# A chunked delta-rule attention in front of two MLPs: the head in another order, and the state's products only where the state is in use

## The reference

```
k_n = k / (norm(k) + 1e-06)
state = zeros(B, H, D, D)
for t in range(S):
    y[t]  = q[t] @ state
    v_old = state applied to k_n[t]
    state = state + beta[t] * outer(k_n[t], v[t] - v_old)
# then: mixture of 8 experts (logits = x_norm @ emb_norm.T / tau, one expert a token),
# then: (relu(x @ w_in) ** 2) @ w_out
```

## Time and profile before

| | us |
|---|---|
| median of 3 runs (1204.06 to 1205.07) | 1204.73 |
| the profiled execution, whole | 1206.8 |
| its span, first to last instruction | 1205.0 |
| attention, until about | 432 |
| experts, until about | 780 |
| last MLP, until the end | 1205 |

### The profile page before, as it was taken

The page is one execution under the profiler, slowest core; times in us unless marked ns, Lnnn a source line. Parts: engine busy times, 40 slices in busy tenths (PEclk is TensorE's granted clock), DMA queues, the critical chain, the costliest instruction groups (busy, mean ns, idle before and its releaser), DMA issues. The chain is left out here.

```text
span 1205.0 us, 24540 instructions
## 1 busy us (share of the span) xinstructions
PE 1131.3 (94%) x10176; PEld 971.6 (81%) x10176; DVE 531.2 (44%) x1216; ACT 441.4 (37%) x1038; POOL 369.8 (31%) x319
## 2 busy tenths in 40 slices
PE   2799999999999889999999999689999999999998
PEld 1588888888888777888778877579999999999997
DVE  4688888788887513211111111043433434343332
ACT  2477777676776511110011100033332323233332
POOL 3566667677777511133451000140010100000000
PEclk9999999999999979999999999989999999999999
DMA  6122223333330369999989640120000000000000
GB/s 109 21 41 39 37 37 68 81 81 81 74 81 16 108 251 349 377 368 375 377 284 335 224 156 27 46 79 1 27 27 27 27 1 27 1 27 1 27 1 27
DMA packets 130558, 130.69 MB, mean 108 GB/s; under 512 B 78280, under 2 KB 116880, under 8 KB 130448
## 3 DMA queue, kind: packets, MB, share of 16 engines
q1 hardware_dynamic: 120448, 105.72, 28.9%
q0 software_dynamic: 5536, 17.31, 4.1%
q10 hardware_dynamic: 4464, 6.10, 1.4%
HBM read 129.70 MB, written 21.43 MB: 125 GB/s over the span
## 5 line engine op out<-in xcount | busy, mean ns | idle before, releaser
L1501 PE MATMUL mlp_ps<-xg_t,win 128*128 128x512 f32 x864 | 216.3, 397 | 1.4 <-DVE xg_t L1574 1.4
L1512 PE MATMUL mlp_ps<-wout,sq_hl 128*128 128x384 f32 x1152 | 215.4, 336 | 0.0
L1512 PEld LDWEIGHTS mlp_ps<-wout,sq_hl 128*128 128x128 f32 x1152 | 204.2, 188 | 7.2
L1501 PEld LDWEIGHTS mlp_ps<-xg_t,win 128*128 128x128 f32 x864 | 161.5, 190 | 32.2 <-DVE xg_t L1574 1.8
L1232 PEld LDWEIGHTS expert_ps<-xs_t,w_sb 128*128 128x128 f32 x1488 | 173.5, 194 | 8.9 <-ACT xs_t L1258 1.0
L1232 PE MATMUL expert_ps<-xs_t,w_sb 128*128 128x128 f32 x1488 | 173.8, 277 | 0.6 <-ACT xs_t L1258 0.6
L1242 PE MATMUL expert_ps<-w_sb,ht_sb 128*128 128x384 f32 x496 | 165.1, 486 | 0.0
L1242 PEld LDWEIGHTS expert_ps<-w_sb,ht_sb 128*128 128x128 f32 x496 | 91.8, 190 | 57.5
L1581 DVE TENSOR_TENSOR sq<-relu 128x512 f32<-128x512 f32 x96 | 66.5, 692 | 160.9 <-ACT relu L1539 154.8
L767 DVE TENSOR_TENSOR p_cur<-newt,cst 128x256 f16<-128x256 f32 x288 | 109.0, 420 | 46.8 <-PE newt L413 43.4
L1539 ACT ACTIVATE relu<-mlp_ps 128x512 f32<-128x512 f32 x96 | 57.3, 597 | 171.9 <-PE mlp_ps L1501 171.5
(11 more groups left out here) (199 smaller groups left out, 1577.2 us busy)
## 6 DMA issues: line engine op xcount, KB each, us to landing
w_sb<-in_moe_w SPq DMA_DIRECT2D x62, 1536.0 KB
xs<-sorted_x SPq DMA_DIRECT2D x31, 192.0 KB
sorted_y<-ys ACTq DMA_DIRECT2D x31, 192.0 KB, 5.9
k_raw<-in_k SPq DMA_DIRECT2D x24, 192.0 KB, 3.0
q_pad<-in_q SPq DMA_DIRECT2D x24, 192.0 KB, 3.9
v_raw<-in_v SPq DMA_DIRECT2D x24, 192.0 KB, 4.1
out<-o_sb SPq DMA_DIRECT2D x6, 768.0 KB, 3.5
sorted_x<-zeros SPq DMA_DIRECT2D x11, 384.0 KB, 5.5
```

The lines of the kernel that those rows point to most:

```text
L1501: mm = pe.matmul(ps[:, 4 + f % 2, :], win[:, a, kd, f * P:(f + 1) * P], xg_t[:, par, b, kd], start=(kd == 0 and a + b == 0), stop=(kd == K ...
L1512: mm = pe.matmul(ps[:, t, 0:DM], sq_hl[:, f % RING, a, t * P:(t + 1) * P], wout[:, b, f], start=(f == 0 and a + b == 0), stop=(f == K2 - 1 ...
```

## The change

- SP issues k of tile 0 first, then the constants and beta; after GpSimd's first fill (q_pad, now its first) come q0, k1, v0, the embedding and tau, q1, v1, and the rest. k, q and v have semaphores of their own. Loads of tiles 4 to 7 wait for `s_d1` (v read by `difference`) instead of `s_r0`.
- The embedding's normalization moves into the loops: `norm_emb` and `root_emb` into turn -1, `scale_emb`, `turn_emb` and `keep_emb` into turn 0 (`scale_emb` in front of `first_t(0)`, `keep_emb` in front of `high_rhs(0)`; the two casts of `count_w` go with it).
- `turn(n, 0)` waits for `k_pad` and q, not for `kb_nat`; `update` waits for `kb_nat`.
- `p_cur` is filled in `norm_k(0)`, and only its odd blocks (half the elements). The state is cleared behind `kb_nat(0)` instead of in front of `kb_nat(1)`.
- For tiles 0 to 3 `start_values`, `old_outputs` and `first_rhs` are left out, and v takes the place of rhs. For tiles 20 to 23 `kb_nat`, `update` and `new_state` are left out. Both leave the result as it is, since the state is zero in the one case and unread in the other.

```diff
@@ sync
+        load_k(0)
         sp.dma_start(cst[:, :], consts).then_inc(s_const, 16)
         sp.dma_start(beta_rows[:, :, :], ...).then_inc(s_beta, 16)
+        sp.wait_ge(s_zero, 1)
+        load_q(0)
+        load_k(1)
+        load_v(0)
         sp.dma_start(emb_rows[:, :], emb).then_inc(s_small, 16)
         sp.dma_start(tau_sb[:, 0:1], ...).then_inc(s_small, 16)
+        load_q(1)
+        load_v(1)
...
+            if n < 2 * B:
+                wait(sp, s_d1, n - 3)
+            else:
+                sp.wait_ge(s_r0, n - 3 - B)
@@ gpsimd
-        pool.memset(rt.zeros[:, :], 0.0)
-        for pad in (q_pad, k_pad):
-            pool.memset(pad[:, :, :, :], 0.0)
+        pool.memset(q_pad[:, :, :, :], 0.0).then_inc(s_zero, 1)
+        pool.memset(k_pad[:, :, :, :], 0.0)
         pool.memset(kb_nat[:, :, :, :], 0.0).then_inc(s_zero, 1)
+        pool.memset(rt.zeros[:, :], 0.0).then_inc(s_zero, 1)
...
-            if n == 0:
-                pool.wait_ge(s_setup, 3)
...
+            if n >= NP - B:
+                return
             wait(pool, s_su_ps, n - 3)
             pool.wait_ge(s_kpad, n + 1)
-            if n == 1:
-                pool.memset(state[:, :, :, :], 0.0).then_inc(s_init, 1)
             pool.tensor_tensor(kb_nat[:, n % B, :, 0:D], ...).then_inc(s_kb, 1)
+            if n == 0:
+                pool.memset(state[:, :, :, :], 0.0).then_inc(s_init, 1)
@@ tensor
             if p == 0:
-                pe.wait_ge(s_kb, n + 1)
+                pe.wait_ge(s_kpad, n + 1)
+                pe.wait_ge(s_q_in[n % B], 16 * (n // B + 1))
@@ tensor: start_values and old_outputs; vector: first_rhs
+            if n < B:
+                return
@@ tensor: update; vector: new_state
-            if not there(n):
+            if not there(n) or n >= NP - B:
@@ scalar: square_k
-            act.wait_ge(s_in[n % B], 48 * (n // B + 1))
+            act.wait_ge(s_k_in[n % B], 16 * (n // B + 1))
@@ scalar: high_rhs
+            if n < B:
+                act.wait_ge(s_v_in[n % B], 16)
+                wait(act, s_x1_ps, n)
+                act.copy(rhs_hi[:, :, :], v_raw[:, n % B]).then_inc(s_rhi, 1)
+                return
@@ scalar: the loop
+            if n == -1:
+                root_emb()
...
             newton_tt(n, 6)
+            if n == 0:
+                keep_emb()
             root(n + 3)
+            if n == -3:
+                keep_beta()
             high_rhs(n)
@@ vector: norm_k
-            if n == 1:
+            if n == 0:
+                dve.wait_ge(s_const, 16)
                 for level in range(1, LEVELS):
-                    ins = dve.tensor_copy(p_cur[:, level - 1], ident.unsqueeze(1).to_broadcast([P, H, P]))
+                    own = odd_blocks(ident.unsqueeze(1), level)
+                    ins = dve.tensor_copy(odd_blocks(p_cur[:, level - 1], level),
+                                          own.to_broadcast([P, H] + list(own.shape[2:])))
@@ vector: the loop
             first_rhs(n - 1)
+            if n == -1:
+                norm_emb()
+            if n == 0:
+                scale_emb()
             first_t(n)
```

More of the change, by code:

```diff
@@ L152, in attention @@
     s_small = sem("s_small")
-    s_in = [sem("s_in0"), sem("s_in1"), sem("s_in2"), sem("s_in3")]
-    s_setup = sem("s_setup")
+    s_k_in = [sem(f"s_k_in{b}") for b in range(4)]
+    s_q_in = [sem(f"s_q_in{b}") for b in range(4)]
+    s_v_in = [sem(f"s_v_in{b}") for b in range(4)]
+    s_beta = sem("s_beta")
+    s_beta_ps = sem("s_beta_ps")
+    s_emb_t = sem("s_emb_t")
+    s_count_w = sem("s_count_w")
     s_zero = sem("s_zero")
@@ L321, in difference @@
             pool.wait_ge(s_x1, n + 1)
-            pool.tensor_tensor(d1[:, :, :], rhs[:, :, :], x1[:, :, :], ALU.subtract).then_inc(s_d1, 1)
+            right = v_raw[:, n % B] if n < B else rhs[:, :, :]
+            pool.tensor_tensor(d1[:, :, :], right, x1[:, :, :], ALU.subtract).then_inc(s_d1, 1)
         def low_part(n):
@@ L437, in start_values @@
                 return
+            if n < B:
+                return
             pe.wait_ge(s_t3, 4 * n + 4)
-            wait(pe, s_state, 2 * n)
+            pe.wait_ge(s_state, 2 * min(n, NP - B))
             for p in range(HP):
@@ L493, in new_outputs @@
             pe.wait_ge(s_u, n + 1)
+            if n < B and hf == 0:
+                wait(pe, s_lg, n)
+                pe.wait_ge(s_emb_t, 1)
             for h in range(4 * hf, 4 * hf + 4):
                 mm = pe.matmul(y_ps[:, h * D:(h + 1) * D], aq[:, n % B, h, P:2 * P], u_all[:, h],
-                               start=False, stop=(h == H - 1), skip_group_check=True)
+                               start=(n < B and h == 0), stop=(h == H - 1), skip_group_check=True)
             if hf == 1:
@@ L550, in _ @@
             route(n - 2)
+            if n == 0:
+                turn_emb()
             newton_p(n, 3)
@@ L707, in reciprocal_norm, with norm_emb, scale_emb @@
             dve.wait_ge(sem_in, base + 5)
[L709 to L717 removed]
+        def norm_emb():
+            dve.wait_ge(s_small, 32)
+            dve.tensor_tensor_reduce(out=y_sq[0:E, :], in0=emb_rows[:, :], in1=emb_rows[:, :], scale=1.0, scalar=0.0,
+                                     op0=ALU.mult, op1=ALU.add, accum_out=emb_n[:, 0:1]).then_inc(s_en, 1)
+            dve.reciprocal(tau_sb[:, 1:2], tau_sb[:, 0:1]).then_inc(s_tau, 1)
+            dve.tensor_copy(rt.base[:, :], cst[:, cs.REGION:cs.REGION + E]).then_inc(rt.s_base, 1)
+        def scale_emb():
+            dve.wait_ge(s_en, 2)
+            reciprocal_norm(emb_n[:, 0:1], emb_n[:, 1:2], [emb_n[:, i:i + 1] for i in (2, 3, 4, 5)], s_en, 2)
+            dve.reciprocal(emb_n[:, 6:7], emb_n[:, 5:6]).then_inc(s_tau, 1)
+            dve.wait_ge(s_tau, 2)
+            dve.tensor_scalar(emb_rows[:, :], emb_rows[:, :], emb_n[:, 6:7], tau_sb[:, 1:2], ALU.mult, ALU.mult)\
+               .then_inc(s_en, 1)
         def sum_k(n):
```

95 lines of the change are left out of this document (51 added, 44 removed).

## The result

The changed kernel took 1194.37 us (median of 4 runs, 1193.41 to 1196.90), the kernel before 1204.90 on the same chip (4 runs): 10.5 us faster, a ratio of 0.991 with an interval from 0.990 to 0.993. The prediction was 1190.8 with a range from 1186 to 1197. The profiled execution took 1194.31 with a span of 1192.5, so the two traces are 12.5 us apart.

The account below looks back on a forecast made before the run. The head was taken as bound by waits across engines, the tiles nearly by TensorE. Head 9.8 us plus tiles and last update 4.1 make 13.9: 1204.73 - 13.9 = 1190.8 us, range 1186 to 1197.

Parts of the forecast that it names:

- k first, table, k_pad: Head, tile 0: k, loaded first, lands at 3.9 us; root's table load follows its square; k_pad starts at 7.4.
- the dearer price: Head: a table switch also drains about 1.38 us, making k_pad and the time 1.4 us later; no chance given.
- The turn: Head, tile 0: no longer waiting for kb_nat, it starts at about 8.6 us instead of 15.70.
- The fills: Head, VectorE: six half copies of p_cur take 4.8 us (ends 2.1 and 6.2); first masking starts at 12.6.
- short fills: Rival, head: the p_cur copies take 2.1 us, first masking at 11.0, time 1189.2 us; chance 0.13.
- The ring: Head, tile 0's four maskings: 3.36 us steps from 12.6, the fourth at 22.7 against 32.84, 10.1 us earlier.
- The scaling of the embedding: Head, VectorE in front of the first transpose: 1.6 us against 1.26 of idle time, 0.3 us late.
- Turn 0 and keep_emb: First tile's turn, ScalarE: keep_emb puts 0.8 us before solve(0); charged 0.3 us (ends 0 and 0.8).
- more stretches at the lower clock: Rival, TensorE's clock: two or three more drops, 2 us for one, time about 1196 us; chance 0.12.
- What is left out: Attention: omitted products give 0.45 us each in turns 1-3, 0.4 in turn 4, 0.3 each in 21-23; last update 1.8.
- the full worth: Rival, tiles: TensorE alone bounds them; products give 7.6 + 2.6 + 1.8 us instead of 4.4, time 1183.2; chance 0.05.
- The slower case: Rival, tiles 1 to 4: TensorE falls to 1.2 GHz and stays; 1225 us with all four so; chance 0.02.

Follow-up runs that it names:

- experiment 8: The changed kernel with turn(0, 0) waiting for kb_nat again; 1194.96 us, ratio 0.991 to the kernel before.
- experiment 1: The changed kernel with scale_emb moved into turn -1, behind the third masking of tile 0, where GpSimd is idle; 1191.07 us, ratio 0.988 to the kernel before.
- experiment 10: The changed kernel run once more, unedited, for a second trace; 1195.79 us.
- experiment 12: The changed kernel with p_cur filled whole again (1024 elements instead of 512) at its new place in norm_k(0); 1196.86 us, ratio 0.992 to the kernel before.
- experiment 7: experiment 1 with the six p_cur fills in two groups of three, in VectorE's waits between tile 0's maskings; 1192.65 us, ratio 0.989 to the kernel before.
- experiment 2: The changed kernel with scale_emb in place, its two 8x1 tensor_tensor instructions written as tensor_scalar; 1194.56 us, ratio 0.991 to the kernel before.
- experiment 6: experiment 1 with 26 extra, unread identity transposes in TensorE's waits of turns -1 and 0; 1191.74 us, ratio 0.989 to the kernel before.
- experiment 5: experiment 1 with keep_emb's casts and copy moved behind store_turned(n + 2, 1), at the end of turn 0; 1192.21 us, ratio 0.989 to the kernel before.
- experiment 9: The kernel before, run once more, unedited, for a second trace; 1208.35 us.
- experiment 11: experiment 7 plus late keep_emb, extra transposes in turns -1, 0 and 1, constants in two loads, k_pad(0) not waiting for constants; 1186.27 us, ratio 0.983 to the kernel before.
- experiment 4: The changed kernel with kb_nat, update and new_state back for tiles 20 to 23; 1195.58 us, ratio 0.991 to the kernel before.
- experiment 3: The changed kernel with start_values, old_outputs and first_rhs back for tiles 0 to 3, loads' waits as before; 1196.78 us, ratio 0.993 to the kernel before.
- the second pair: Second traces of the kernel before and the changed kernel, both rerun unedited; 1208.35 and 1195.79 us.

## Why the prediction was near, point by point

*k first, table, k_pad.* Right: 3.52 and 7.02 us for 3.9 and 7.4. The load of 192 KB, first in the queue, was squared 2.8 us behind its issue, a little below the low end of the earlier trace rows. The table's load took 1.28 us (4.06 to 5.34) and the root followed at 5.35: the dearer price would have put k_pad beyond 8. The Trainium skill (ScalarE: Activation LUTs, What ACT_TABLE_LOAD costs) adds a drain of 1.38 us to a switch; this row shows none. In nine of the eleven later traces with the changed head k_pad was released by the constants and not by the norm, at 7.00 to 7.99.

*The turn.* Right in time (7.90 for 8.6), but the part of it that came from the removed wait is worth little: 0.3 us at most by experiment 8. The bound of the ring's start is fills and constants. The constants' landing (6.8 us here at the latest, up to 7.9) is a term that the prediction's sum did not have; where they land later, the fills and the whole ring move with them (masking at 12.90 in experiment 1). The cover of 1.2 us for q0 was too large: in experiments 10 and 12 the turn waited for q0, and only the fills hid it.

*The fills.* Right: 4.66 us for 4.8. The choice to stay near the old stretch, since GpSimd is at work beside them, was the right one; "short fills" (2.1 us) is refuted for this place and true for another (2.2 us in experiment 7).

*The ring.* Right: 3.35 us steps, four of them, the fourth masking at 21.86 for 22.7.

*The scaling of the embedding.* This is the step that failed: "1.6 against 1.26 of idle time: 0.3 late" was 2.9 late. Its durations had been taken from a stretch in which GpSimd was idle, and it was moved beside `tt_cur` and `a_l`, two of GpSimd's three longest instructions. Experiments 1 and 2 show the cause. For the fills the same neighbour had been priced, for the scaling it had not, since its instructions are so small; but the length of a hold is that of the other engine's instruction, not of one's own. The head gave 8.1 us and not 9.8. That the time still came near owes something to luck: the ring started 0.8 us earlier than predicted, and turns 2 to 4 gave 0.4 more.

*Turn 0 and keep_emb.* keep_emb cost 0.2 us and in a second trace 0.4, for 0.3. But turns 0 and 1 lost 1.7 us: 0.95 in turn 0, where the clock rose 13.3 us behind the first Newton product instead of 7.5, and 0.7 in turn 1, where a drop lasted 6.9 us instead of 3.4. This is the rival "more stretches at the lower clock", in the one place where the forecast had none. The length of turn 0 goes with that rise in every trace, whatever the kernel: 14.1 us where the clock was up at the first product (experiment 6), 15.5 to 15.8 where it rose about 5 to 6 us behind it (5, 8, 9, 11), 16.1 at 7.5, 17.1 to 17.6 from about 13 on (the rest). Experiment 5 differs from experiment 1 by nothing that runs before the rise, experiment 8 from the changed kernel by one wait, and yet the rise came some 8 us sooner in both: executions of the same code can differ in it. The sum of turns 0 and 1 was 31.96 and 32.04 us before and 33.62 and 35.02 after; in experiment 4, whose turns 0 and 1 are the changed kernel's, it is 34.15, and in the others from 30.42 to 33.65. Whether leaving out the products has a part in this is open: turn 0 is as long with them (experiment 3), but turn 1 had no drop there. Experiment 6 shows that the rise follows, at least there, what TensorE does in its waits, but not which pause it is that the change made worse, if it is one. What decides where the clock rises and falls here stays open.

*What is left out.* Right: turns 2 to 4 gave 0.58, 0.57 and 0.52 us for 0.45, 0.45 and 0.4, and GpSimd is the next bound; the full worth is refuted. Turns 21 and 22 gave 0.5 for 0.6 in this pair of traces, but nothing in the second pair (31.07 and 31.05 us), and experiment 4 could not confirm them. The end (turn 23 and the last update) gave 2.1 to 2.2 us for 0.3 + 1.8, and 2.8 in the second pair. Together these terms were predicted at 2.7 and measured at 2.6, 2.8 and, by experiment 4, 2.2: the update's eight matmuls and GpSimd's and VectorE's parts are gone at half clock, and between old_outputs and new_outputs no weights are loaded any more.

*The sum.* 13.9 us were predicted for the profiled pair. Counted by the prediction's own terms it is 8.1 + 1.7 + 0.5 + 2.1 - 1.7 = 10.7, and the medians give 10.5. The head gave 1.7 less than predicted (scaling 2.6 less, the ring's start 0.8 more), turns 0 and 1 gave -1.7 where -0.3 + 0.45 were predicted, and turns 2 to 4 0.4 more. These are the 3.2 us between 13.9 and 10.7; the medians missed by 3.6.

The slower case, a low clock without end, didn't come: from 55.1 us to the end of the attention the clock was full, with TensorE busy for 13.7 of 15.1 us.

## What to carry to other kernels

Before a small VectorE instruction is moved into a gap, look at what GpSimd does in that gap: here 0.15 us became 2 us, and a term taken from a stretch with GpSimd idle was wrong by 2.6 us, more than the 2.1 of one GpSimd instruction. A product left out of a nearly full engine gives only the time to the next bound (0.5 of 1.9 us a tile here), and a removed wait only what the next one leaves (0.3 at most, of 1.8). Where the clock moves in the stretch that a change touches, read its effect from the stages, since two executions of one kernel differ there by more than the edit.

## What the runs showed of the hardware

GpSimd's tensor instructions and clearings hold some VectorE instructions and not others. Held to the end of the GpSimd instruction: a tensor_tensor of 8x1 (0.15 to 2.04 us), a tensor_scalar of 8x384 (0.47 to 2.41), casts of 128x512 (0.37 to 2.37). Not held, beside the same instructions: reciprocals and tensor_scalars of 8x1 (0.13 to 0.20), also with a scalar column as second operand, and maskings, which read PSUM. The Trainium skill (SBUF — State Buffer, SBUF: two separate sides) describes this as an exclusive lock on a pair of ports: whichever of a VectorE instruction in a two-port mode or with two SBUF inputs and a GpSimd instruction starts first keeps it for its whole length (with two SBUF inputs only against a GpSimd instruction that reads SBUF). The traces agree, with 29.46 us beside 29.45; which instructions run in a two-port mode they do not show. The prediction did not use it.

TensorE's clock rose 7.5 and 5.5 us behind the first Newton product in the two traces of the kernel before, and in those with the changed head some 12.5 to 14 us in seven (13.3 in the first), 4.8 in two (experiments 5 and 8), 22.8 in one (experiment 4) and 5.8 with extra transposes (experiment 11). It was up at the first product where TensorE had been busy for 9.05 of the 9.87 us before it (experiment 6). TensorE was busy for 13.1 of the 13.3 us before the rise in the changed kernel.

SyncE's queue took 0.4 to 0.6 us each to issue the first five loads of the changed kernel, but 2.53 us for the sixth, the first v, and 0.3 to 1.4 for those behind it. In experiment 11 the first v took 1.20 and a later k 2.79.
